# Fetching the first block of a weight product early, and moving one pair's preparation into the next stage

## The reference

```
for t in range(S):
    cur = np.einsum('bhd,bhe->bhde', u[None] * kt, vt)
    y[:, :, t] = np.einsum('bhd,bhde->bhe', rt, state + cur)
    state = wt[:, :, :, None] * state + np.einsum('bhd,bhe->bhde', kt, vt)
...
x = (((x @ w1) * (x @ w2)) @ w3) @ w_out
...
logits = x @ w_gate
noise_scale = np.log1p(np.exp(x @ w_noise))
noisy_logits = logits + noise_scale * noise
top2 = np.argpartition(-noisy_logits, 2, axis=1)[:, :2]
out[mask] += top2_w[mask, k, None] * (np.maximum(x[mask] @ w1[e], 0.0) @ w2[e])
```

## Time and profile before

| what | value |
|---|---|
| time, median of 3 (lowest, highest) | 1007.42 us (1006.35, 1007.83) |
| the profiled execution | 1000.34 us, its span 998.6 us |
| mean granted TensorE clock | 0.988 of full |
| TensorE busy | 958.8 us, 96% of the span |
| VectorE busy | 685.1 us, 69% |
| ScalarE busy | 526.9 us, 53% |
| GpSimd busy | 223.9 us, 22% |

### The profile page before, as it was taken

How to read it: one execution, slowest core, us unless ns; L and a number is a source line. 1 busy time by engine, 2 the same in 40 slices (tenths; PEclk the granted TensorE clock), 3 DMA queues, 4 the chain that set the end, 5 groups by cost and what they waited for, 6 DMA issues and landing times.

```text
span 998.6 us, 18069 instructions
## 1 busy us (share of the span) xinstructions
PE 958.8 (96%) x6825; PEld 902.6 (90%) x6825; DVE 685.1 (69%) x1145; ACT 526.9 (53%) x986; POOL 223.9 (22%) x209
## 2 busy tenths in 40 slices
PE   4898999999999999999999999999999999999995
PEld 3555899999999999999999999999999999999995
DVE  7788786969797878263778585765857658576570
ACT  2543444445454635234545575665756657566560
POOL 0000100020202020203344323333332332323321
PEclk9998999999999999999999999999999999999998
DMA  8985524253435220306348797877968779787751
GB/s 257 281 252 159 169 80 133 87 180 94 130 103 172 73 70 29 101 1 220 115 169 264 198 298 210 245 255 210 304 206 246 253 213 299 207 246 254 211 158 16
DMA packets 87308, 179.02 MB, mean 179 GB/s; under 512 B 18915, under 2 KB 44261, under 8 KB 87221
## 3 DMA queue, kind: packets, MB, share of 16 engines
q1 hardware_dynamic: 73844, 157.18, 49.5%
q0 software_dynamic: 12976, 20.66, 9.9%
q10 hardware_dynamic: 400, 0.02, 0.0%
HBM read 152.22 MB, written 26.97 MB: 179 GB/s over the span
## 4 chain that ended last, share of the span: by engine, by line
PE 87%; DVE 7%; ACT 3%; issue 2%; POOL 0%; DVEq 0%; POOLq 0%; ACTq 0%
PE bank L1214 20%; PE pp L1230 20%; PE bank L785 11%; PE bank L802 7%; PE fx L785 6%; PE fx L802 4%; PE yu L1273 3%; PE pp L186 3%; DVE kdiv L258 2%; PE tr L1195 2%; PE yu L1255 1%; PE fx L1255 1%; PE fx L672 1%; PE yu L207 1%; PE yu L230 1%
## 5 line engine op out<-in xcount | busy, mean ns | idle before, releaser
L1123 POOL DMA_INDIRECT result<-x2s,who x55 | 92.9, 1689 | 284.5 <-ACT x2s L1347 265.2
L1334 DVE SCALAR_TENSOR_TENSOR abl<-bank,abh 128x512 fp32r<-128x512 f32 x96 | 66.2, 691 | 109.9 <-ACT abh L1329 109.9
L974 POOL DMA_INDIRECT slot_entry<-entry,slot_i x48 | 52.0, 1082 | 345.0 <-DVE token_f L963 332.9
L1214 PE MATMUL bank<-xh,set_up_h 128*128 128x256 f32 x384 | 109.2, 284 | 0.0
L1214 PE MATMUL bank<-xh,set_up_l 128*128 128x256 f32 x384 | 108.6, 283 | 0.0
L1214 PE MATMUL bank<-xl,set_up_h 128*128 128x256 f32 x384 | 108.6, 283 | 0.0
L1329 ACT ACTIVATE abh<-bank 128x512 fp32r<-128x512 f32 x96 | 57.5, 599 | 81.6 <-PE bank L1214 81.4
L312 ACT ACTIVATE att<-ident,diag 128x128 f32<-128x128 f32 x192 | 60.6, 392 | 69.5 <-DVE diag L297 69.5
L785 PE MATMUL bank<-xh,w12h 128*128 128x384 f32 x264 | 89.6, 339 | 1.7 <-DVE xl L481 1.5
L785 PE MATMUL bank<-xh,w12l 128*128 128x384 f32 x264 | 88.4, 335 | 0.0
L785 PE MATMUL bank<-xl,w12h 128*128 128x384 f32 x264 | 88.2, 334 | 0.0
(11 more groups left out here) (260 smaller groups left out, 2654.5 us busy)
## 6 DMA issues: line engine op xcount, KB each, us to landing
up_raw<-in_moe_w SPq DMA_DIRECT2D x93, 512.0 KB, 4.6
down_raw<-in_moe_w SPq DMA_DIRECT2D x124, 384.0 KB, 4.7
vs<-in_v_rows SPq DMA_DIRECT2D x16, 384.0 KB, 3.7
wt<-in_w SPq DMA_DIRECT2D x32, 144.0 KB, 2.9
kt<-in_k SPq DMA_DIRECT2D x32, 144.0 KB, 3.0
rt<-in_r SPq DMA_DIRECT2D x32, 144.0 KB, 3.4
kn<-in_k_rows SPq DMA_DIRECT2D x16, 288.0 KB, 2.9
rn<-in_r_rows SPq DMA_DIRECT2D x16, 288.0 KB, 3.5
```

The costliest lines, as they stand in the source:

```text
L974: nc.gpsimd.indirect_dma_start(slot_entry, bass.IndirectOffsetOnAxis(slot_i[:, s, n:n + 1], 0), entry[:, s, n, :], None).then_inc(scattere ...
L1123: nc.gpsimd.indirect_dma_start(out, bass.IndirectOffsetOnAxis(who[v % 4][:, s, 0:1], 0), yo[v % 2][:, s, 0:DM], None, bounds_check=N - 1, ...
L1214: last = nc.tensor.matmul(bank[m % 2][:, f * T2:(f + 1) * T2], wp[:, kk, c:c + P], xp[:, kk, :], start=(n == 0), stop=(n == 3 * KD - 1))
L1334: nc.vector.scalar_tensor_tensor(hl[:, 2 * m:2 * m + 2, :].rearrange("p a t -> p (a t)"), bank[m % 2][:, :], 0.0, hh[:, 2 * m:2 * m + 2, : ...
```

## The change

1. Block 0 of w3 is fetched right after the first decays, before `w_out`, and its `w3_mm` steps go over the 384 columns of `w_out` alone: two steps after the first three `wo_turn` steps, two after the other three. They no longer wait for `wo_ready`. The 16 gate columns of block 0 are a step of their own, `gates_mm`, after `gates_turn`.
2. `wo_gates` and `gates_turn` use the bank `yu` in place of `fx`, and ScalarE in place of VectorE copies the 16 columns into `wo`.
3. In stage one the steps of pair 4 (batch 1's first) are taken out of the slots (`own_slots`) and the last two slots dropped: `[:TAIL - 10]` with `TAIL = 8` is `[:-2]`. 38 slots are left, of 43.
4. The round of batch 0 in stage two begins with `first_slots()`, the preparation of that pair, and has 47 slots in place of 40. The other rounds keep their order.

```diff
-TAIL = 3
+TAIL = 8
...
+        def own_slots(slots, pairs):
+
+            return [[step for step in slot if step[1] < pairs] for slot in slots]
...
-            front = [("wo_turn", n, 0) for n in range(6)] + [("wo_gates", 0, 0), ("gates_turn", 0, 0)]
-            build = [("w3_mm", n, quarter) for n in range(KF) for quarter in range(4)]
-            front, build = front + build[:3], build[3:]
+            front = []
+            for part in range(2):
+                front += [("wo_turn", KD * part + kk, 0) for kk in range(KD)]
+                front += [("w3_mm", 0, 2 * part + n) for n in range(2)]
+            front += [("wo_gates", 0, 0), ("gates_turn", 0, 0), ("gates_mm", 0, 0)]
+            build = [("w3_mm", n, quarter) for n in range(1, KF) for quarter in range(4)]
             order = threaded(front, first_slots())
-            order += threaded(build, [slot for q in range(HP) for slot in pair_slots(q, q == 0)] + [[]] * TAIL)
+            order += threaded(build, own_slots([slot for q in range(HP) for slot in pair_slots(q, q == 0)], HP)[:TAIL - 10])
...
                 sp_input_load(sp, 0, 0, 0)
+                load_w3(0)
                 for part in range(2):
...
                 for n in (1, 2):
                     sp_input_load(sp, 0, 0, n)
-                load_w3(0)
...
-                        nc.scalar.copy(gates_side[:, :], fx[:, 0:2 * P]).then_inc(gates_out, 1)
+                        nc.scalar.copy(gates_side[:, :], yu[:, 0:2 * P]).then_inc(gates_out, 1)
+                    elif step == "gates_turn":
+                        act.wait_ge(gates_full, 2)
+                        nc.scalar.copy(wo[:, :, DM:WA].rearrange("p (j t) e -> p t j e", t=2),
+                                       yu[:, 2 * P:4 * P].rearrange("p (t j e) -> p t j e", t=2, j=4)[:, :, :, 0:2 * E]
+                                       ).then_inc(wo_ready, 1)
...
                     elif step == "w3_mm":
+                        columns = WA if q else DM
                         if n == 0:
                             pe.wait_ge(w3_loaded[q % 2], 16 * (q // 2 + 1))
-                            pe.wait_ge(wo_ready, 1)
                             need(pe, wal_ready, q - 1)
...
+                    elif step == "gates_mm":
+                        pe.wait_ge(wo_ready, 1)
+                        for m in range(KF):
+                            last = nc.tensor.matmul(sums[0][:, DM:WA], w3T[0][:, m, :], wo[:, m, DM:WA],
+                                                    start=(m == 0), stop=(m == KF - 1))
+                        last.then_inc(wa_full, 1)
...
-            both = threaded(group_steps(False), [slot for q in range(HP) for slot in pair_slots(q)])
+            every_slot = [slot for q in range(HP) for slot in pair_slots(q)]
+            both = [threaded(group_steps(False), first_slots() + every_slot if b == 0 else every_slot) for b in range(B - 1)]
```

More of the change, by code:

```diff
@@ L42 @@
 LENGTH = {"up": 6, "down": 6, "turn": 0, "route": 0, "place": 0,
-          "wo_turn": 2, "wo_gates": 5, "gates_turn": 1, "w3_mm": 5}
+          "wo_turn": 2, "wo_gates": 5, "gates_turn": 1, "w3_mm": 5, "gates_mm": 1}
 def need(eng, sem, count):
@@ L540, in first_sp @@
                 for step, q, n in order:
-                    if step == "w3_mm" and n == 3:
+                    if step == "gates_mm" or step == "w3_mm" and n == 3 and q:
                         if q + 2 < KF:
@@ L581, in first_act @@
                         nc.scalar.copy(w12h[:, m, kk, :], wraw[(q - 1) % 2][:, :]).then_inc(w12h_ready, 1)
-                    elif step == "w3_mm" and n == 3:
+                    elif step == "gates_mm" or step == "w3_mm" and n == 3 and q:
                         act.wait_ge(wa_full, q + 1)
@@ L618, in first_dve @@
                     dve_attention(dve, 0, step, q, n)
[L619 to L624 removed]
+                    if step == "w3_mm" and n == 2 and 1 <= q <= 2 * KD:
                         m, kk = divmod(q - 1, KD)
@@ L1458, in rest_sp @@
                 for b in range(B - 1):
-                    for step, q, n in both:
+                    for step, q, n in both[b]:
                         if step == "down" and n == DOWNS - 1:
```

14 lines of the change are left out of this document (4 added, 10 removed).

## The result

| | kernel before | changed kernel |
|---|---|---|
| median (lowest to highest) | 1007.62 us (1006.35 to 1008.55), 4 runs | 1023.98 us (1023.11 to 1025.92), 4 runs |
| profiled execution, span | 1000.34 us, 998.6 us | 1024.39 us, 1022.7 us |
| TensorE busy | 958.8 us, 96% | 968.1 us, 95% |

The ratio is 1.0166, 95% interval 1.0147 to 1.0185: slower by 16.4 us, where +9.2 was forecast. The time is above the upper end of the range, 1021.0.

What follows compares the result with a forecast made beforehand. TensorE was taken to bound stage two, and before that whatever releases stage two's first product. Terms 4.3 + 1.8 - 2.5 + 1.6 + 3.2 + 0.8 = +9.2 us on 1007.4 gave 1016.6 us, range 1011.0 to 1021.0.

Steps and rivals of the forecast that it cites:

- A: Front of stage one: first score delayed because ScalarE's gate copies stand behind spreads, then 16 small records; +4.3 us.
- F: Rest of batch 0's round: 47 slots share the steps of 40 and VectorE is 92% busy, small waits; +0.8 us.
- C: Tail of stage one: batch 1's preparation leaves it, so the load of `tokens` sets its length; -2.5 us.
- B: Pairs of stage one: the low halves of w1 and w2 move among the chain's operations; +1.8 us.
- D: Score and keys of batch 1's first pair move from a wait to behind eight `up` steps; +1.6 us.
- E: Head of stage two: TensorE waits for mask 0 while VectorE does the moved preparation; +3.2 us.
- clock in the round: Half clock behind the stalls of batch 0's round: no term in the sum, 0 us.
- the list of what would show it: For the front: first L186 at 29 to 31 us, TensorE waiting for ScalarE's copy into `wo`, L312 in two sixes.
- rival 3: Clock falls more in `gates_mm`, behind the head's stall and in the tail: +14.1 us, 1021.5 us; chance 0.13.
- rival 2: No stall at the head of stage two, VectorE's waits overlapping more: +6.0 us, 1013.4 us; chance 0.13.
- rival 4: Full clock all through stage one and no stall at stage two's head: +2.3 us, 1009.7 us; chance 0.07.
- rival 5: Early block pays in full, first score at 21.1 us: +0.1, 1007.5 us, or 1004.3 without head stall; chance 0.05.

Runs made afterwards that it cites:

- c2_before: The kernel before, unchanged, run again for its profile beside the changed kernel; its median on that chip was 1002.36 us.
- c4_before: The kernel before, unchanged, run a second time for one more profile on that same chip; median there 1002.36 us.
- e7_empty_slots: The kernel before with seven empty slots ahead of batch 0's round and nothing else; ratio 1.0050 to the kernel before.
- e6_filler: The changed kernel plus unused products, eight ending stage one and 16 ahead of batch 1's first pair's second score; ratio 1.0135 to the kernel before.
- e3_gates_first: The changed kernel with the gate copies ahead of the first pair's spreads in ScalarE's queue, `gates_mm` behind them; ratio 1.0101 to the kernel before.
- e9_front_spreads_filler: Kernel before plus early block 0, gate copies ahead of spreads, batch 1's first pair's twelve spreads heading batch 0's round, five unused products ending stage one; ratio 0.9979.
- c0_before: The kernel before, unchanged, run once more for a second profile; ratio 1.0005, profiled execution 1001.62 us.

## Why the prediction was off, step by step

The direction and the places were right; the size was not: +9.2 forecast, +16.4 measured (+17.7 between profiled executions of one chip). The step that failed first is the clock: the sum has nothing for half clock behind the stalls of batch 0's round, without a reason, and the runs showed 3.9 us. Behind it come the half clock in the front (A, 2.9 us too low), the narrower slots (F, 1.6 too low, and put down to the wrong cause) and the tail (C, 1.8 off).

The terms, in the profiles, add up to 18.9 of the landmark's +19.4. Against c2_before and c4_before the landmark is only 16.8 and 17.1 us later. The profile ahead of the prediction was a quick one: full clock at the head of stage two (1.5 us) and the fourth pair's mask 0 at 84.22, where the three later ones have 85.00 to 85.47.

| step | forecast | measured | read from |
|---|---|---|---|
| A, the front | +4.3 | +7.2 | second mask 37.11 against 29.89 |
| B, the pairs | +1.8 | +1.3 | fourth pair's mask 0 at 92.70, +8.5, less 7.2 |
| C, the tail | -2.5 | -0.7 | 114.50 - 92.70 = 21.8 against 22.5 |
| D, score and keys moved | +1.6 | +1.6 | durations unchanged; e7_empty_slots |
| E, stall at the head | +3.2 | +3.2 | the wait for L320 in 100 to 250 us |
| F, rest of the round | +0.8 | +2.4 | small waits 1.3 + 0.8 + 0.3; e7_empty_slots: 4.2 - 1.6 = 2.6 |
| clock in the round | 0 | +3.9 | e6_filler |

**A.** The score was forecast at 29.4 plus a share of half clock and came at 30.72, within the list of what would show it. The step that failed is where the half clock was let end: "at half clock for 3 us the 16 records take 3.4 us". They took 3.59, but the clock, at half since 25.6 us, came back only at 35.8, and the first score, the keys and four records of the next block, all on the chain, ran at half speed too: 0.7 + 0.6 + 1.2 = 2.5 us. e3_gates_first, which has neither, shows that this and the wait behind ScalarE are all of A; e9_front_spreads_filler shows that the half clock can come without that wait. The price per small record was right: 0.12 us at full clock, as the transposes of the earlier trace rows have it. The Trainium skill's 25 ns for a small product ("TensorE: Matmul & The Clock Gate", section "Wait — 56ns, not 53.3ns?") are a floor. These records, float32 with weights of 128 x 128, stay far above it, at 120 ns each, so that the estimate of 0.4 us made from it was no price for them.

**B and C.** B was 0.5 too high. C had the choice between full clock and half clock and took the middle, 20.0; it was the upper end, 21.8 against 21.5 reckoned.

**D and E** came out as reckoned. That D is the moved score and keys is borne out by the rounds with full clock at the head: 94.2 to 94.3 us where they stand behind the first `up` steps, 92.3 to 92.5 where they do not. E is the longest count in the prediction, some twenty operations on two engines, and it met the trace to 0.1 us, in part by luck. TensorE was ready for the second score 17.4 us after the first product and got it at 20.6, where the count has 15.7 and 18.9: half clock at the head, which the count left out, moved both ends by 1.7 us.

**F** was put at VectorE's load, with "no idle of over 1 us". One wait is 1.3 us, and e7_empty_slots, which leaves that load as it was, has the same. The cause is the order: 47 slots on the same steps are narrower, and two `spread` slots then stand ahead of the copy that frees a bank. I had the order at hand and counted only its head.

**The clock in the round** was in the sum with nothing, and in rival 3 with 1.5. It is the largest error. (Against c2_before and c4_before, which lose 1.5 us to half clock at the same place, the change's own share is 2.4.) TensorE idles for 6.05 us ahead of the first `up` product, and for 3.2 at the head; with each there goes a stretch at half clock (0.53 in 114 to 118, 0.57 in 134 to 142 us), and e6_filler shows the price, 3.9 us. Rival 3 named these places and gave 1021.5, still 2.5 us under the median; its chance of 0.13 was too small. The rows that it gives for the low windows, are ScalarE's; the windows are in the earlier trace rows. The Trainium skill says that idle TensorE brings the half clock back ("TensorE: Matmul & The Clock Gate", section "HAM oscillation — how this bites in real kernels"). This case's trace agrees at 25.6, 111 and 135 us, with waits of 2.70, 6.05 and 3.23 us; in e9_front_spreads_filler the clock falls at 25.0 us with no wait of over 0.5 us since 10.4.

Rivals 2, 4 and 5 each needed something that did not occur: no head stall, full clock, the first score at about 21 us. But rival 5's idea lives in another form: with ScalarE's order mended, the first score came at 24.55 to 26.11, mostly ahead of the 25.92 to 27.56 of the old front, though block 0 is then whole and TensorE starts its transposes some 2 us later.

## What to carry over

When a change makes TensorE wait, as here for 2.7, 3.2 or 6.0 us, count the wait and also what runs behind it at half clock on the chain: here that was 2.5 us in the front and 3.9 in the round.

Where steps are spread evenly among slots, more slots also narrow those that are left alone. An experiment with empty slots prices that by itself, here, with the move of score and keys, at 4.2 us of a round's 11.7.

Work moved from an engine's critical stretch gains only up to the next thing in its queue. Here that was 1 us, and the slot that it was moved in cost 1.8 until it shared the slot of the score.

## What the hardware showed that was not expected

The half clock in the front lasted 10.2 us (25.6 to 35.8), though TensorE was busy without a break from 27.2, on 16-column products for the first 3.6. I had read it in 20 to 22 us, behind 3.69 us of waiting, and took it for a matter of some 3 us; in four of the nine profiles with the old front it lasts until about 26 us. What ended it is not settled.

The kernel before has a half clock at the head of stage two in some profiled executions (0.62 and 0.58 in 108 to 112 us in c2_before and c4_before) and not in others (1.00 in the profile of before and in c0_before). The idle time ahead of the first `up` product is 1.83 and 1.87 us in the first two, 1.55 and 1.73 in the others; four profiles are too few to make a rule of it.

In the finale ScalarE stands still for 4.3 to 4.5 us, for 3.1 us, or both, with no releaser in the profile. Of the 11 profiles taken where the kernel before had a median of about 1002 us none has it; of the 8 taken where that was 1007 to 1008 us, seven have. The eighth is the profile of before, whose execution took 1000.34 us where its runs took 1006 to 1008. What makes these waits is open.
